# Two-stage attention opening: first q and k loaded by pairs of heads, and transposed pooled probabilities copied out by another engine

## The reference

```python
def _attn_ref(q, k, v):
    q_d = q.reshape(B, H, Sd, factor, D).mean(axis=3)   # factor = 4; k_d, v_d alike
    out_up = np.repeat(sm_attn(q_d, k_d, v_d), factor, axis=2)
    mask = np.abs(pos[:, None] - pos[None, :]) < factor
    scores = np.where(mask, scale * np.matmul(q, k.transpose(0, 1, 3, 2)), -1000000000.0)
    ...
    return out_up + np.matmul(attn, v)

x = attn_out.transpose(0, 2, 1, 3).reshape(B * S, H * D)
x = _moe_ref(x=x, **moe_kwargs)        # 8 experts, each token to one, 288 tokens each
return _moe2_ref(x=x, **moe2_kwargs)   # (2304, 512) -> 2048 -> 512
```

## Times and profile before

| | us |
|---|---|
| median of 3 runs | 904.61 |
| the runs | 904.27 to 905.18 |
| the profiled execution | 906.95 |
| its span, first to last instruction | 905.2 |
| TensorE busy (its weight loads) | 850.5 (757.4) |
| VectorE busy | 623.8 |
| ScalarE busy | 328.6 |
| GpSimd busy | 145.4 |

### The profile page before, as it was taken

One profiled execution on the slowest core, in us unless ns is written; L12 is line 12 of the kernel. 1 busy time (PEld: TensorE's weight loads), 2 busy tenths in 40 slices (PEclk: granted clock), 3 DMA queues, 4 the chain that ended last, 5 costly groups with the idle time before them and its releaser, 6 DMA issues.

```text
span 905.2 us, 19231 instructions
## 1 busy us (share of the span) xinstructions
PE 850.5 (94%) x7220; PEld 757.4 (84%) x7220; DVE 623.8 (69%) x1683; ACT 328.6 (36%) x1041; POOL 145.4 (16%) x186
## 2 busy tenths in 40 slices
PE   7999999962799999999999999999999999999996
PEld 6677878661798899899889889998898899899995
DVE  5485858458889967876786567667867966875332
ACT  2757787733453242142133112421431242143111
POOL 4654646310100100110020001100200110010001
PEclk9889999975799999999999999999999999999998
DMA  7667571034652420340142021303300430340000
GB/s 163 147 160 188 125 168 46 19 80 126 192 183 81 126 94 1 115 129 2 47 125 74 1 73 60 117 1 95 119 29 1 142 101 2 93 152 1 1 1 35
DMA packets 122676, 77.27 MB, mean 85 GB/s; under 512 B 64280, under 2 KB 105240, under 8 KB 122584
## 3 DMA queue, kind: packets, MB, share of 16 engines
q1 hardware_dynamic: 119416, 65.83, 26.3%
q0 software_dynamic: 3168, 10.23, 3.6%
HBM read 66.59 MB, written 9.44 MB: 84 GB/s over the span
## 4 chain that ended last, share of the span: by engine, by line
PE 67%; DVE 8%; issue 1%; ACT 0%; POOL 0%; DVEq 0%; ACTq 0%; POOLq 0%
PE banks L967 21%; PE banks L968 19%; PE banks L969 19%; PE banks L988 2%; PE banks L972 2%; PE banks L973 1%; DVE neg L1364 1%; PE banks L976 1%; PE banks L1017 1%; DVE w1s L1444 1%; DVE wout L1444 1%; DVE onehot L1317 1%; DVE win L1444 1%; DVE act L1366 0%; DVE hid L1372 0%
## 5 line engine op out<-in xcount | busy, mean ns | idle before, releaser
L1546 ACT CAST hid<-act 128x256 fp32r<-128x256 f32 (+1 forms) x128 | 55.5, 434 | 335.5 <-DVE act L1366 335.4
L967 PE MATMUL banks<-xy,win 128*128 128x256 f32 (+1 forms) x448 | 136.2, 304 | 2.1 <-DVE act L1366 2.1
L969 PE MATMUL banks<-xy,win 128*128 128x256 f32 (+1 forms) x448 | 132.7, 296 | 0.0
L968 PE MATMUL banks<-xy,win 128*128 128x256 f32 (+1 forms) x448 | 132.6, 296 | 0.0
L1364 DVE TENSOR_SCALAR neg<-banks,alph 128x256 f32<-128x256 f32 (+1 forms) x128 | 66.1, 516 | 90.1 <-PE banks L969 75.9
L967 PE MATMUL banks<-wout,hid 128*128 128x512 f32 x288 | 116.9, 406 | 0.4 <-DVE hid L1372 0.4
L968 PE MATMUL banks<-wout,hid 128*128 128x512 f32 x288 | 113.5, 394 | 0.0
L969 PE MATMUL banks<-wout,hid 128*128 128x512 f32 x288 | 112.8, 392 | 0.0
L1581 POOL DMA_INDIRECT rows<-x_rows,id_new x24 | 23.6, 981 | 500.9 <-DVE id_new L1325 496.0
L554 ACT ACTIVATE prob<-banks,nbias 96x102 f32<-96x102 f32 (+1 forms) x256 | 85.9, 350 | 15.9 <-DVE nbias L474 8.1
L967 PEld LDWEIGHTS banks<-xy,win 128*128 128x128 f32 x448 | 85.3, 191 | 6.1 <-DVE act L1366 3.1
(11 more groups left out here) (216 smaller groups left out, 1865.0 us busy)
## 6 DMA issues: line engine op xcount, KB each, us to landing
raw<-in_moe_w SPq DMA_DIRECT2D x128, 256.0 KB, 3.7
qn<-in_q SPq DMA_DIRECT2D x48, 96.0 KB, 2.6
kn<-in_k SPq DMA_DIRECT2D x48, 96.0 KB, 2.5
vn<-in_v SPq DMA_DIRECT2D x8, 576.0 KB
x_rows<-xs SPq DMA_DIRECT2D x24, 192.0 KB, 2.3
raw<-in_moe_w_in SPq DMA_DIRECT2D x16, 256.0 KB, 3.6
raw<-in_moe_w_out SPq DMA_DIRECT2D x16, 256.0 KB, 3.4
vw<-in_v SPq DMA_DIRECT2D x16, 204.0 KB
```

The costliest lines, as they stand in the source:

```text
L967: nc.tensor.matmul(out_ap, a_hi, b_hi, start=start, stop=False)
L968: nc.tensor.matmul(out_ap, a_lo, b_hi, start=False, stop=False)
L969: return nc.tensor.matmul(out_ap, a_hi, b_lo, start=False, stop=stop)
L1546: nc.scalar.copy(hid[:, (FC + j) % 3, 0, 0:CHUNK[k]], act[:, j % 2, 0:CHUNK[k]]).then_inc(h_hi, 1)
```

## The change

Seven edits:

1. **Loads.** q and k of batch 0 come by pairs of heads, 48 transfers of 96 rows x 2 heads (`load_first_qk`) in place of 24 of 96 rows x 4 heads. Each pair's q and each pair's k has a semaphore of its own. The first half of v goes ahead of the last pair.
2. **Order of the opening.** One pair in each of the turns -3 to 0. In turn 0 the flip comes first, before the last pair. In turns -3 to 0 `max` stands before `normalize`. The second half of v is summed in turn 0 and not in turn -1.
3. **Windows.** Each window of v is loaded by two transfers, 96 rows and the 6 (or 3) that are left.
4. **Copies.** `pdT` is copied out by VectorE, in all 16 pooled units (two copies each).
5. **Dense matmuls** for the units 0 to 5 and not only 2 to 5; 9 fillers at the start and not 18.
6. **GpSimd**: `ones` right after the identity tiles, then the masks, then the routing's constants.
7. The first local scores also wait, by name, for the last q and k copies.

```diff
-            first = {-LAG: (0, 1), 1 - LAG: (2,), 2 - LAG: (3,)}.get(t, ())
-            for hp in first:
-                qk(0, hp, all_four)
+            if t == 0:
+                self.steps += [("flip", t, 0), ("flip", t, 1)]
+            if t + LAG < HP:
+                qk(0, t + LAG, all_four)
...
-            if 0 <= t < NU:
+            if 0 < t < NU:
                 self.steps += [("flip", t, 0), ("flip", t, 1)]
+            if t <= 0:
+                self.steps.append(("max", t + LAG, 0))
...
-            if t in (1 - LAG, 2 - LAG):
-                self.steps += [("pool_v", 0, 3 * (t + LAG - 1) + stage) for stage in range(3)]
-            if 0 <= t + LAG < NU:
+            if t in (1 - LAG, 3 - LAG):
+                self.steps += [("pool_v", 0, 3 * (t + LAG - 1) // 2 + stage) for stage in range(3)]
+            if 0 < t and t + LAG < NU:
                 self.steps.append(("max", t + LAG, 0))
...
-                self.who.append("act" if items[u][0] == "pooled" else "dve")
+                self.who.append("dve")
...
+    def load_first_qk(e, hp):
+
+        heads = slice(2 * hp, 2 * hp + 2)
+        for t, (dst, src) in enumerate(((qn, q), (kn, k))):
+            for r in range(R):
+                e.dma_start(dst[:, r, heads], src[0, heads, r * T:(r + 1) * T].rearrange("h p d -> p h d")
+                            ).then_inc(qk_first[t][hp], 16)
...
-            s0 = j * T - PAD + lo
-            e.dma_start(vw[lo:hi, b % 2, j, :].rearrange("p (h d) -> p h d", h=H),
-                        vt[b, s0:s0 + hi - lo]).then_inc(vw_in[b % 2], 16)
+            for a, z in ((lo, lo + T), (lo + T, hi)):
+                e.dma_start(vw[a:z, b % 2, j, :].rearrange("p (h d) -> p h d", h=H),
+                            vt[b, j * T - PAD + a:j * T - PAD + z]).then_inc(vw_in[b % 2], 16)
...
-        load_qk(e, 0, 0)
-        load_qk(e, 0, 1)
+        for hp in range(HP - 1):
+            load_first_qk(e, hp)
         load_v(e, 0, 0)
+        load_first_qk(e, HP - 1)
         load_v(e, 0, 1)
...
-        if (t, c) == (0, 0) and hp % (HP // 2) == 0:
-            e.wait_ge(qk_in[hp // (HP // 2)], 16 * 2 * R * (b + 1))
+        if b == 0 and c == 0:
+            e.wait_ge(qk_first[t][hp], 16 * R)
+        elif (t, c) == (0, 0) and hp % (HP // 2) == 0:
+            e.wait_ge(qk_in[hp // (HP // 2)], 16 * 2 * R * b)
...
-            e.wait_ge(consts["fixed_made"], consts["ones_at"])
-        if 2 <= u <= LAG + 2:
+            e.wait_ge(consts["ones_made"], 1)
+        if u <= LAG + 2:
             pe_dense(psum[:, 512 * 7:512 * 8], 3)
...
             if u == HP:
+                for c in range(2):
+                    wait_emptied(e, "qk", 0, (1, HP - 1, c))
                 e.wait_ge(masks_made, 1)
...
-        pe_fill(pF[0], 18)
+        pe_fill(pF[0], 9)
...
+            elif kind == "flip":
+                e.wait_ge(flipped, PLAN.flipped("flip", u, x))
+                if ITEMS[u][2] >= 2:
+
+                    e.wait_ge(flipped, PLAN.flipped("apply", u - 2, 0))
+                nc.vector.tensor_copy(pdT[:, u % 2, x].rearrange("p r m -> p (r m)"),
+                               pF[PLAN.place["flip", u, x] % RING][0:HALF, 0:2 * SD]).then_inc(emptied_dve, 1)
```

More of the change, by code:

```diff
@@ L165, in attention @@
     qk_in = [sem("qk_in0"), sem("qk_in1")]
+    qk_first = [[sem(f"{t}_first{hp}") for hp in range(HP)] for t in "qk"]
     vn_in, wg_in = [sem("vn_in0"), sem("vn_in1")], sem("wg_in")
@@ L378, in pe_apply @@
             if x == 0:
-                e.wait_ge(vw_in[b % 2], 16 * NT * (b // 2 + 1))
+                e.wait_ge(vw_in[b % 2], 16 * 2 * NT * (b // 2 + 1))
             e.wait_ge(summed, b * NT + x)
@@ L562, in scalar @@
         for kind, u, x in STEPS:
-            pooled = kind in ("flip", "apply") and ITEMS[u][0] == "pooled"
+            pooled = kind == "apply" and ITEMS[u][0] == "pooled"
             if kind == "qk" and x[2] == 1:
@@ L567, in scalar @@
                 act_exp(e, u)
[L568 to L574, removed]
             elif kind == "apply" and pooled:
@@ L616, in pool_norm, with gpsimd @@
             nc.gpsimd.tensor_tensor(p, p, inv.unsqueeze(2).to_broadcast([rows, heads, width]), ALU.mult).then_inc(normed, 1)
-    def gpsimd(e):
+    def gpsimd(e, make_fixed):
         band = consts["pool_steps"]
@@ L635, in gpsimd @@
         nc.gpsimd.memset(consts["spare"][:], 0.0).then_inc(masks_made, 1)
+        make_fixed(e)
         for kind, u, x in STEPS:
@@ L678, in make_route_consts @@
     g.iota(f["row_at"][:, 2, :], pattern=[[0, E]], base=1, channel_multiplier=1, allow_small_or_imprecise_dtypes=True).then_inc(made, 1)
-    n, tiles, at, cut_at = 8, NT * T // TILE // B, 0, 0
-    for t in ("ones", "segment", "before"):
+    n, tiles, at, cut_at = 7, NT * T // TILE // B, 0, 0
+    for t in ("segment", "before"):
         g.memset(f[t][:], 1.0).then_inc(made, 1)
@@ L1675, in attention_then_experts @@
     NT = B * S // T
-    N_CONSTS = 12 + len(set(DIGIT_BITS)) + 2 * B
+    N_CONSTS = 11 + len(set(DIGIT_BITS)) + 2 * B
     with ExitStack() as whole, ExitStack() as first:
@@ L1696, in attention_then_experts @@
         psum = [banks[:, 512 * i:512 * (i + 1)] for i in range(8)]
-        ident_made, fixed_made = sem("ident_made"), sem("fixed_made")
+        ident_made, ones_made, fixed_made = sem("ident_made"), sem("ones_made"), sem("fixed_made")
         consts = dict(ident=ident, ident16=ident16, spare=spare, made=ident_made, n_made=4,
-                      ones=fixed["ones"], fixed_made=fixed_made, ones_at=8,
+                      ones=fixed["ones"], ones_made=ones_made,
                       pool_steps=sem("mask_steps"))
@@ L1748, in _ @@
                 n += 1
-            make_route_consts(nc, e, fixed, T, NT, E, J, TILE, SLOTS, B, fixed_made)
-            attn["gpsimd"](e)
+            nc.gpsimd.memset(fixed["ones"][:], 1.0).then_inc(ones_made, 1)
+            attn["gpsimd"](e, lambda e: make_route_consts(nc, e, fixed, T, NT, E, J, TILE, SLOTS, B, fixed_made))
             moe["gpsimd"](e)
```

## The result

The changed kernel takes 908.1 us (median of 8 runs, 907.3 to 910.2) against 904.9 for the kernel before on the same chip: ratio 1.0036, interval 1.0021 to 1.0051. It is 3.2 us slower, where 3.0 us faster was forecast. Against more runs of before (104 executions beside the experiments, median 905.3) it is 2.8. One execution of before, 915.9 us and in the slower state, is left out everywhere.

A forecast was written before the change was run, and what follows sets the result against it. Opening bound in turn by transfers, a serial chain per pair and a 4.05 us ScalarE-VectorE loop, with half clock from 38 to 50 us. Terms -3.4 + 0.9 - 0.5 = -3.0 from 904.6 gave 901.6, range 898.8 to 907.0.

The forecast's parts named there:

- Price of a 48 KB transfer: SyncE's first loads: 0.47 us start to start, an estimate between 0.41 and 0.52.
- a rival at 904: Opening loads: a 48 KB transfer costs as much as 96 KB, 0.52 us; chance 0.22 shared with little effect.
- Arrivals: Opening: pair 0's k lands at 8.4 us, pairs follow 5.6 apart, pair 3's k at 25.8; landing takes 2.4.
- Chain behind a pair: Opening, last pair: 4.0 us from k's landing to the end of its scores, so unit 3's end at 29.8.
- From there: From unit 3's scores at 29.8 to unit 4's exponentials at 35.05, against 33.46 before, so 1.6 us behind.
- a turn: Loop between ScalarE and VectorE from unit 4 on: 4.05 us each time round, unchanged by the edits.
- Does it stay up?: TensorE's clock: no idle stretch over 0.5 us from 29 to 41, the 1.30 us one goes; opening gaps 1.2.
- the rival of a clock that falls there: Opening: waiting for pairs halves the clock, +4.0 us on the last pair, 905.6 to 909, said 908; chance 0.14.
- Where the sum starts: Unit 8's scores end at 47.3, not 50.66: -3.4 us if the clock stays up; sum taken from median 904.6.
- Batch 1's q and k: Next batch's loads, behind the windows: land at about 42 us, not 40.7, TensorE wants them at 41.0; charged +0.9.
- Copies: 32 copies of 0.409 us leave ScalarE; 0.1 to 0.2 a batch in batches 1 to 3, counted -0.5.
- marks that I set: Right: 12 issues 5.6 us, unit 4 near 35, unit 8 near 48. Wrong: 6.2, early half clock, late reciprocal.

The follow-up runs named there:

- e6: Changed kernel with each pair's q and k loaded by one 144 KB transfer a head, 4 a pair instead of 12: 902.0 us.
- e4: Changed kernel with the first half of v (576 KB) moved behind the last pair of heads: 913.3 us.
- e2: Kernel before with only the windows' edit, each loaded as 96 rows and a rest of 3 or 6: 905.4 us.
- e12: Kernel before with batch 0's q and k in one 144 KB transfer a head, pair after pair, and pdT copies on VectorE: 901.5 us.
- e5: Changed kernel with the 32 pdT copies put back on ScalarE: 910.2 us.
- e1: Kernel before with only the copies' edit, VectorE making the 32 pdT copies: 905.1 us.
- e11: Kernel before with 144 KB loads of batch 0's q and k, pdT copies on VectorE and windows in two parts: 900.7 us.
- e13: Changed kernel with 144 KB loads of q and k, one a head, and pdT copies back on ScalarE: 903.7 us.

## Why the prediction was wrong, point by point

**Price of a 48 KB transfer:** 0.49, between the 0.47 taken and the upper bound of 0.52. Over 35 transfers this is 0.8 us. The rule of the Trainium skill (DMA: Bandwidth & Descriptors, Rules for kernel authors: coalesce, under 64 KB is mostly overhead) was weighed as a rival at 904. On the issuing side this case's rows bear it out: 0.49, 0.52 and 0.53 us for 48, 96 and 144 KB, the last for the eight transfers of the first two pairs, so an issue costs nearly the same at three times the bytes as long as the bytes do not back up. Going the rule's way, to 144 KB, was worth 6.1 us (changed to e6).

**Arrivals:** k of pair 0 at 8.50 (forecast 8.4) was right, and so was the landing of 2.4 for the first two pairs (2.3 for their last transfers). Pair 2's k was not: 22.17 where the same sum gives 19.7. Of the 2.5, 0.8 are the pitch and 1.6 the landing, 4.0 with the 576 KB of v right behind (e4 without it: 2.4 at most). Pair 3's k, forecast for 25.8, has landed by 27.6. With the 4.0 behind it that would give 31.6, so late arrivals alone do not explain where unit 3's scores end, 34.81.

**Chain behind a pair, the step that failed.** 4.0 from landing to the end of the scores is right at full clock: pair 1, 14.42 to 18.38. But I applied it to pair 3 alone, as if pair 3 waited for its transfers only. It waits for TensorE and VectorE to be done with pair 2 first: its k lay there for 3.4 us. e6 has the price of that: 6.5 us from one pair's scores to the next with the flips between, whatever has landed. From pair 2's k on, then: 22.17 + 5.6 (4.0 stretched by half clock) = 27.75, and 7.1 more to 34.81. I had 29.8. The 5.0 us are 2.5 of late k, 1.6 of half clock, and 1.0 in the last step, for which my numbers left 6.1 (29.8 - 19.7 - 4.0): too little even at full clock.

**From there** to unit 4's exponentials 5.03 (forecast 5.25), and 4.04 a turn (4.05): right.

**Does it stay up?** From 37 to 50 yes, as said. My reason was that the later start does away with the 1.30 us idle stretch of the earlier trace rows. But in the traces of e2 and e12 that wait is there (1.29, 1.31) and the clock stays at 1.00, so the reason is not borne out; what the runs do show is that the copies, for which I counted no clock, raise its mean. In the opening I had gaps of 1.2 us a pair; one was 2.6, and the rival of a clock that falls there, given 0.14, is what happened. The size of the gap is not all of it, as in e5's trace the clock was at half from 14 us, ahead of pair 2. Its place was right, its price (4.0 us on the last pair) too high, since the clock was back at 31: it cost 1.6 and some 0.6 of the last step (7.1 against e6's 6.5).

**Where the sum starts.** I took 3.4 us for the end of the slow stretch off the median of the runs, as a difference of spans. But the stretch was read from one execution whose mean clock was 0.963; 104 executions have 0.9695 on average. Only what the average execution has can be won: by the slope 2.5 us, with e6's 0.9744.

**Batch 1's q and k,** +0.9: the terms that I name give 40.0 (23.9 + 6.4 + 0.9 for the gate's weights + 6.2 + 2.5) and not 42, so the charge did not follow from them. They landed at 45.9, as the windows took 9.0 us and not 6.4, and TensorE, late itself, waits 0.41 for them. **Copies,** -0.5: right for batches 1 to 3 (e1's advance is 0.5 shorter than e2's), but their clock was not in the sum. **Windows,** nothing: right beside late loads (e2), but 1.2 of level beside early ones (e12 to e11). GpSimd's order and the semaphores were not run alone.

Of the marks that I set, the right ones that failed are unit 4 near 35 and unit 8's scores near 48; of the wrong ones, the clock at 0.50 before 35 came true, and so did the late reciprocal: in the last pooled unit of each batch it starts 1.40 us behind the exponentials and not 0.33. The first 12 issues took 5.8 us, between the marks of 5.6 and 6.2.

## What to carry to other kernels

Cut a first load by what the first step needs, but count the issues: here one transfer costs 0.5 us of its queue from 48 to 144 KB, so the first pairs took 2.1 us to issue in 4 transfers and 5.9 in 12, and the last pair's k was there by 19.5 us and not by 27.6. When work is cut into pieces that each wait for the last, walk the chain through every piece with full loads as well; the last arrival alone does not bound it. And where the clock swings, read the stretch that you want to win in the mean of many runs before taking it off their median, and look for the short copy that stands behind long work on a busy engine. Before you call a wait the cause of a slow clock, look for a run that has the same wait and no slow clock.

## What the runs showed of the hardware

- SyncE's pitch per transfer, start to start: 0.49 us for 48 KB in 192 pieces, 0.52 for 96 KB in 384, 0.53 for the first eight of 144 KB in 576. Behind those the pitch grows, 0.64 to 0.75 and once 2.71 us (e6).
- 48 KB transfers moved 99 GB/s (changed, 2 to 18 us), 144 KB transfers 201 GB/s (e6, 4 to 8 us).
- A transfer of 48 KB of the first three pairs lands 1.8 to 2.3 us after its issue, and the one with 576 KB issued right behind it 4.0. One of 144 KB lands after 2.8 us at first and 8.8 at last.
- Executions of the kernel before have mean clocks of 0.962 to 0.976, which is a difference of 25 us at half clock (0.014 x 905 x 2). The 12 us from 38 to 50 at half clock lower the mean by 0.0066 (12 x 0.5 / 905), by the slope 3.4 us.
- In e13 TensorE was busy 3.50 of 5.00 us from 37 to 42 at 1.00, and had 0.50 from 42.2 on though it was busy throughout. In e2 it was busy 3.51 of 5.00 us in the same stretch, with the same wait, and had 1.00 from 42 to 50.
